# Turning the next pair's key and query groups earlier in a pair of heads, with copies counted head by head and the zero fill in portions

## The chip, the cores and the metric

The kernel runs on one core of one Trainium2 chip. The metric is the device time of one execution in microseconds (us); lower is better. The median of three runs stands for the kernel.

## The reference, cut to what matters

Three stages follow each other: an attention, a mixture of experts with one expert per token, and a gated dense layer. The change lies in the attention alone.

```python
# q, k, v: batch 4, heads 8, sequence 1152, head width 64
q_pool = q.reshape(B, H, S // 2, 2, D).mean(axis=3)          # 576 queries per head
scores = scale * np.matmul(q_pool, k.transpose(0, 1, 3, 2))  # 576 x 1152
scores = scores - np.max(scores, axis=-1, keepdims=True)
attn = np.exp(scores)
attn = attn / (np.sum(attn, axis=-1, keepdims=True) + 1e-09)
attn_out = np.matmul(attn, v)
# then: rows of all heads -> 2304 tokens x 512 -> experts -> dense layer
```

## The kernel before

The attention works on 16 pairs of heads, numbered 0 to 15 (`LAST` is 15). The body of a pair is a list of 27 units, `UNITS`, that every engine walks through in the same order, with one program per engine and semaphores between them. The names of the units: "b" and "c" turn and multiply the probabilities of the pair before (second head, and the rest tile of both heads), "a" those of this pair's first head, "x" turns finished output, and "g" (four groups, g0 to g3) turns keys and summed queries of the **next** pair. Three tables say after which unit the scores, the maxima and the exponentials of each of nine query tiles are placed: `SCORES_AT`, `MAXIMA_AT`, `EXP_AT`. Tile 0 of the next pair is handled at units 24 to 26 of this one.

On PE (TensorE) a unit is first a *fill*, four 128x128 transposes into one of three PSUM banks `ps_t` (L686), and then the *products* of the unit three places earlier (L753, or L762 for "c"). Scores are L784 and, for the last key chunk, L797. The DVE (VectorE) takes the maxima and writes the low part of every turned bank; ACT (ScalarE) writes the high part and the exponentials.

Keys and queries of a pair take this way. SP (SyncE) loads `raw_k` and `raw_q` (L275, L280, L283); POOL (GpSimd) adds the query pairs into `q_sum` (L405, L413); PE turns them in g0 to g3; ACT and DVE write the parts into `kept_rows`; SP copies these by six DMAs, three for each head, into `kq_t` (L295, L296, L298), the operand of the scores. There is one `raw_k`, one `raw_q` and one `parts` buffer, so SP works in a fixed order. Its procedure `next_pair(p)` waits until the DVE has finished g3 of pair p, copies the parts for pair p+1, and then loads keys, queries and values of pair p+2. I call the start of these copies **T(p)**. Before g0 of pair p+1, PE waits for `kq_loaded` and `q_summed` of pair p+2. Before the first scores of a pair it waits for `kq_copied`, which counts all six copies; ACT waits for it too before it overwrites `parts` in g0.

The lines that say this, with SP's order around them:

```python
sp.wait_ge(t_free, upto(p, kind, every, LAST_G))      # next_pair: g3 is done
copy_parts(1 - par)
if load:
    load_kq(p + 2)
    sp.wait_ge(v_split, p + 2)
    load_v(p + 2)
...
pe.wait_ge(kq_loaded, 16 * KQ_DMAS * (p + 2))         # PE, before g0 of pair p
pe.wait_ge(q_summed, 2 * (p + 2))
```

SP also fills with zeros the rows that the expert stage scatters into: `xs_dram` (25 tiles of 128 rows, 6400 KB) and the tail of `ys_dram` (7 tiles, 1792 KB), both before the first `next_pair`.

Of the kernel before, what the change touches and what calls it, by code (L numbers as in the profile page):

```python
# [4 lines left out]
F32 = mybir.dt.float32  # L5
# [7 lines left out]
P = 128  # L13
# [48 lines left out]
def attention(nc, q, k, v, w_gate, w_out_gate, w1, x_dram, xs_dram, ys_dram, shared):  # L62
# [17 lines left out]
    B, H, SK, D = k.shape  # L80
    SQ = SK // 2
    E = w_gate.shape[1]
    PAIRS = B * H // 2
# [31 lines left out]
    ]  # L115
    SCORES_AT = [(25, 26), (0, 1), (2, 3), (6, 7), (10, 12), (12, 14), (16, 16), (19, 20), (22, 23)]
    MAXIMA_AT = [(24, 25), (0, 0), (3, 3), (5, 7), (11, 12), (13, 14), (16, 16), (18, 19), (20, 22)]
    EXP_AT = [(0, 0, 1), (2, 3, 4), (5, 5, 7), (9, 11, 12), (13, 13, 13), (16, 16, 16), (18, 19, 20), (21, 21, 22), (24, 25, 25)]
# [54 lines left out]
    with ctx:  # L173
# [6 lines left out]
        def sem(name):  # L180
            return ctx.enter_context(nc.semaphore(name))
# [30 lines left out]
        ys_zeroed = sem("ys_zeroed")  # L212
# [7 lines left out]
        kq_copied = sem("kq_copied")  # L220
# [21 lines left out]
        KQ_DMAS, X_DMAS, COPIES = 6, 3, 6  # L242
# [26 lines left out]
        with nc.Block() as block:  # L269

            @block.sync
            def _(sp):
# [18 lines left out]
                def copy_parts(par):  # L291

                    for h in range(2):
                        src, at = parts[h * D:h * D + D].bitcast(F32), h * HEAD
                        sp.dma_start(kq_t[par][0:D, at:at + HEAD].bitcast(F32), src[:, 0:LO_K]).then_inc(kq_copied, 16)  # L295
                        sp.dma_start(kq_t[par][D:P, at:at + CH * P].bitcast(F32), src[:, LO_K:LO_K + CH * P]  # L296
                                     ).then_inc(kq_copied, 16)
                        sp.dma_start(kq_t[par][D:P, at + CH * P:at + HEAD].bitcast(F32), src[:, CH * P:LO_K]  # L298
                                     ).then_inc(kq_copied, 16)
# [16 lines left out]
                def next_pair(p, par, kind, load=True):  # L316
# [3 lines left out]
                    if load:  # L320
# [15 lines left out]

                sp.wait_ge(zeros_ready, 1)
                n = xs_dram.shape[0] // P
                sp.dma_start(xs_dram.rearrange("(t p) d -> p t d", p=P),
                             zeros[:, :].rearrange("p (o d) -> p o d", o=1).broadcast_to([P, n, 512])  # L340
                             ).then_inc(x_stored, 16)

                tokens = x_dram.shape[0]
                sp.dma_start(ys_dram[tokens:, :].rearrange("(t p) d -> p t d", p=P),
                             zeros[:, :].rearrange("p (o d) -> p o d", o=1).broadcast_to([P, n - tokens // P, 512])
                             ).then_inc(ys_zeroed, 16)
                next_pair(0, 0, "first")
                with sp.Fori(1, LAST - 2, 2) as p:
                    next_pair(p, 1, "mid")
                    store(p - 1, "mid")  # L350
                    next_pair(p + 1, 0, "mid")
                    store(p, "mid")
                next_pair(LAST - 2, 1, "mid")
# [14 lines left out]
                sp.wait_ge(kq_copied, 16 * COPIES * PAIRS)  # L368
# [4 lines left out]
                sp.wait_ge(ys_zeroed, 16)  # L373
# [109 lines left out]
            def _(act):  # L483
# [6 lines left out]
                def take(p, par, kind, j, step):  # L490
# [4 lines left out]
                    if is_group(step):  # L495
                        if step[1] == 0:

                            act.wait_ge(kq_copied, 16 * COPIES * (p + 1))
                        group_hi(step[1], ring(kind, j))
                        return  # L500
# [182 lines left out]
            def _(pe):  # L683
# [89 lines left out]
                def scores(p, par, tile, h, opening=False):  # L773
# [4 lines left out]
                    if tile == 0 and h == 0:  # L778

                        pe.wait_ge(kq_copied, 16 * COPIES * (p + 1))  # L780
# [1055 lines left out]
```

## Time and profile before

| what | value |
|---|---|
| median of 3 runs | 1724.21 us (1719.8 to 1727.47) |
| the profiled execution, its own time | 1722.07 us |
| its span, first to last instruction | 1720.3 us |
| mean granted TensorE clock | 0.911 of full |
| busy share of the span | PE 83%, PE weight loads 72%, DVE 51%, ACT 37%, POOL 20% |
| end of the attention's last product on PE | 852.5 us from the span's start |

The 1.8 us between span and time lie around the program. The attention takes the first half of the span; the busy shares are averages over stages that differ, so they say little about one of them.

### The profile page before, as it was taken

Reading aid. Unit: us, or ns where it says so; the run is one execution under the profiler, and the core shown is the slowest. Engines: PE = TensorE matmul, PEld = TensorE weight load, DVE = VectorE, ACT = ScalarE, POOL = GpSimd, SP = SyncE. Lnnn points to the kernel's source line nnn. Section 1 sums busy time; section 2 is a strip of 40 time slices with the busy share of each in tenths; the row PEclk is TensorE's granted clock in tenths of the full one; section 3 lists DMA queues with packets and bytes.
Section 4 is the critical chain, followed back from the end, with each engine's and each line's share of the span. In section 5 each row is a group of like instructions: output and inputs, shape, how many; then the busy total and the mean of one; then the engine's idle time right before and its main releaser. Section 6 shows DMA issues by size and latency. Waiting matters only on the chain. (4 is left out here: it accounts for less than half of the span.)

```text
span 1720.3 us, 24853 instructions
## 1 busy us (share of the span) xinstructions
PE 1433.4 (83%) x7733; PEld 1236.4 (72%) x7734; DVE 871.5 (51%) x1658; ACT 639.0 (37%) x1549; POOL 345.1 (20%) x241
## 2 busy tenths in 40 slices
PE   2688777778777778877848988999999999999998
PEld 1567655667655666665636767878789999999998
DVE  1477555667655567656674434444464323323232
ACT  1466555566555466555542133010053111111111
POOL 3011101111101111101078278030130101010000
PEclk7689888889888889888978989999999999999999
DMA  8723444432344432246156356131152001000000
GB/s 208 227 48 75 92 106 106 106 67 65 80 106 106 106 80 65 67 106 182 29 199 240 105 205 219 43 104 37 55 158 87 31 7 38 24 12 18 0 19 19
DMA packets 127738, 156.85 MB, mean 91 GB/s; under 512 B 47440, under 2 KB 86352, under 8 KB 125648
## 3 DMA queue, kind: packets, MB, share of 16 engines
q1 hardware_dynamic: 111776, 114.35, 26.4%
q10 hardware_dynamic: 12880, 31.99, 5.5%
q0 software_dynamic: 3040, 9.96, 1.8%
q8 instruction: 25, 0.41, 0.1%
q14 instruction: 17, 0.14, 0.0%
HBM read 87.33 MB, written 29.10 MB: 68 GB/s over the span
## 5 line engine op out<-in xcount | busy, mean ns | idle before, releaser
L784 PE MATMUL ps_s<-kq_t 128*128 128x512 f32 x640 | 228.7, 455 | 171.0 <-DMA kq_t<-kept_rows 163.9
L570 DVE TENSOR_REDUCE maxima<-ps_s 128x1 f32<-128x512 f32 x288 | 194.7, 685 | 241.3 <-PE ps_s L784 240.9
L506 ACT ACTIVATE p_hi<-ps_t 128x512 fp32r<-128x512 f32 (+1 forms) x336 | 193.6, 584 | 229.2 <-PE ps_t L686 225.2
L784 PEld LDWEIGHTS ps_s<-kq_t 128*128 128x128 f32 x640 | 124.9, 214 | 207.5 <-issue 154.4
L649 DVE TENSOR_TENSOR p_lo<-ps_t,p_hi 128x512 fp32r<-128x512 f32 (+1 forms) x336 | 215.0, 666 | 14.0 <-ACT p_hi L506 9.3
L686 PE MATMUL ps_t<-ident,probs 128*128 128x128 f32 x1296 | 207.5, 286 | 0.0
L686 PEld LDWEIGHTS ps_t<-ident,probs 128*128 128x128 f32 x1296 | 171.8, 149 | 46.6 <-issue 6.3
L530 ACT ACTIVATE probs<-ps_s,neg_max 128x512 f32<-128x512 f32 x288 | 198.5, 689 | 17.5 <-DVE neg_max L583 9.8
L1018 POOL TENSOR_TENSOR w_parts<-raw_w,w_parts 128x1024 fp32r<-128x1024 f32 x64 | 150.8, 2392 | 189.2 <-ACT w_parts L1088 189.0
L1634 ACT ACTIVATE silu<-ps_g 128x384 f32<-128x384 f32 x72 | 35.4, 492 | 314.0 <-PE ps_g L1740 314.0
L753 PE MATMUL ps_o<-p_hi,v_hl 128*128 128x512 f32 x288 | 148.1, 514 | 1.9 <-DVE o_sb L590 1.9
L1088 ACT ACTIVATE w_parts<-raw_w 128x1024 fp32r<-128x1024 f32 x64 | 67.0, 1058 | 220.0 <-PE ps_h L1415 104.3
L1687 DVE TENSOR_TENSOR silu<-ps_g,silu 128x384 f32<-128x384 f32 x72 | 40.1, 557 | 210.1 <-ACT silu L1634 210.1
L753 PE MATMUL ps_o<-p_lo,v_hl 128*128 128x512 f32 x288 | 121.0, 420 | 0.0
L397 POOL TENSOR_TENSOR v_hl<-raw_v,zeros 128x1152 fp32r<-128x1152 f32 x16 | 42.4, 2651 | 318.8 <-PE ps_o L762 295.6
L1738 PE MATMUL ps_g<-mxt_hi,wg 128*128 128x384 f32 x288 | 97.5, 339 | 2.4 <-DVE mxt_lo L1662 2.4
L1740 PE MATMUL ps_g<-mxt_hi,wg 128*128 128x384 f32 x288 | 97.7, 339 | 0.0
L1739 PE MATMUL ps_g<-mxt_lo,wg 128*128 128x384 f32 x288 | 97.3, 338 | 0.0
L1738 PE MATMUL ps_v<-mxt_hi,wv 128*128 128x384 f32 x288 | 96.4, 335 | 0.0
L1739 PE MATMUL ps_v<-mxt_lo,wv 128*128 128x384 f32 x288 | 96.4, 335 | 0.0
L1740 PE MATMUL ps_v<-mxt_hi,wv 128*128 128x384 f32 x288 | 96.4, 335 | 0.0
L1413 PE MATMUL ps_h<-w_parts,xst_hi 128*128 x200 | 82.7, 413 | 14.9 <-POOL w_parts L1018 12.1
(190 smaller groups left out, 2851.8 us busy)
## 6 DMA issues: line engine op xcount, KB each, us to landing
raw_w<-in_moe_w ACTq DMA_DIRECT2D x61, 512.0 KB, 3.6
kq_t<-kept_rows SPq DMA_DIRECT2D x32, 608.0 KB, 6.2
kq_t<-kept_rows SPq DMA_DIRECT2D x32, 320.0 KB, 7.1
raw_k<-in_k SPq DMA_DIRECT2D x32, 288.0 KB, 5.4
raw_v<-in_v SPq DMA_DIRECT2D x16, 576.0 KB, 5.4
kq_t<-kept_rows SPq DMA_DIRECT2D x32, 288.0 KB, 6.5
raw_q<-in_q SPq DMA_DIRECT2D x32, 256.0 KB, 4.1
x_by_slot<-zeros SPq DMA_DIRECT2D x1, 6400.0 KB, 21.6
```

The source lines that it names most:

```text
L506: nc.scalar.activation(p_hi[prob_ring(kind, m)][:, 0:w], T[ring(kind, j)][:, 0:w], ACT.Copy).then_inc(hi_ready, 1)
L530: nc.scalar.activation(probs[:, at:at + 512], S[(2 * tile + h) % SR][:, :], ACT.Exp, bias=neg_max[:, tile:tile + 1], accum_out=sums[par][: ...
L570: nc.vector.reduce_max(maxima[:, 3 * tile + h:3 * tile + h + 1], S[(2 * tile + h) % SR][:, :], AX).then_inc(max_done, 1)
L649: nc.vector.tensor_tensor(p_lo[n][:, 0:w], t[:, 0:w], p_hi[n][:, 0:w].bitcast(F32), ALU.subtract).then_inc(t_free, 1)
L686: last = nc.tensor.transpose(dst[:, n * P:(n + 1) * P], src, ident[:, :])
L753: last = nc.tensor.matmul(O[:, :], v_hl[v_par][:, c * P:(c + 1) * P], part[:, :], start=(i == 0 and n == 0), stop=(i == CH - 1 and n == 1))
L784: last = nc.tensor.matmul(S[(2 * tile + h) % SR][:, :], w, kq_t[par][:, at:at + 512], start=(n == 0), stop=(n == len(ops) - 1))
L1018: nc.gpsimd.tensor_tensor(w_part(n, parity, 1, at, PIECE), raw[j % RAW][:, :], w_part(n, parity, 0, at, PIECE).bitcast(F32), ALU.subtract) ...
L1413: nc.tensor.matmul(HB[h][:, :], xh, dyn(0, base, 0, at), start=(c == 0), stop=False)
L1738: nc.tensor.matmul(dst, wh, xh, start=(c == 0), stop=False)
L1739: nc.tensor.matmul(dst, wh, xl, start=False, stop=False)
L1740: last = nc.tensor.matmul(dst, wl, xh, start=False, stop=(c == DC - 1))
```

## The change

It has four parts. (1) `UNITS` is reordered: g1, g2 and g3 move from places 13, 19 and 20 to 10, 13 and 15; the "x" units and the first "a" units come behind g3. The three tables of tiles are rewritten to go with it. (2) `kq_copied` becomes two semaphores, one for each head; PE waits for the first before tile 0 and for the second before tile 4 (`QT`), ACT still for both. (3) The fill of `xs_dram` is cut into one tile and then two tiles per pair, issued by SP behind each store of the loop; the fill of `ys_dram` follows the loop. (4) The first `next_pair` stands ahead of all zero fill.

```diff
--- before.py
+++ after.py
@@ -110,12 +110,12 @@
 
     UNITS = [
         ("g", 0), ("b", 0), ("b", 1), ("b", 2), ("b", 3), ("b", 4), ("b", 5), ("b", 6), ("b", 7),
-        ("b", 8), ("c", 0), ("c", 1), ("c", 2), ("g", 1), ("x", 0), ("a", 0), ("x", 1), ("a", 1),
-        ("a", 2), ("g", 2), ("g", 3), ("a", 3), ("a", 4), ("a", 5), ("a", 6), ("a", 7), ("a", 8),
+        ("b", 8), ("g", 1), ("c", 0), ("c", 1), ("g", 2), ("c", 2), ("g", 3), ("a", 0), ("a", 1),
+        ("x", 0), ("x", 1), ("a", 2), ("a", 3), ("a", 4), ("a", 5), ("a", 6), ("a", 7), ("a", 8),
     ]
-    SCORES_AT = [(25, 26), (0, 1), (2, 3), (6, 7), (10, 12), (12, 14), (16, 16), (19, 20), (22, 23)]
-    MAXIMA_AT = [(24, 25), (0, 0), (3, 3), (5, 7), (11, 12), (13, 14), (16, 16), (18, 19), (20, 22)]
-    EXP_AT = [(0, 0, 1), (2, 3, 4), (5, 5, 7), (9, 11, 12), (13, 13, 13), (16, 16, 16), (18, 19, 20), (21, 21, 22), (24, 25, 25)]
+    SCORES_AT = [(25, 26), (2, 3), (5, 6), (8, 9), (12, 13), (14, 16), (18, 18), (21, 22), (24, 24)]
+    MAXIMA_AT = [(25, 26), (2, 2), (4, 6), (8, 9), (11, 12), (14, 15), (17, 18), (20, 21), (22, 23)]
+    EXP_AT = [(2, 3, 3), (5, 6, 6), (8, 9, 9), (11, 12, 13), (14, 15, 15), (18, 19, 19), (20, 21, 22), (22, 23, 24), (25, 25, 26)]
 
     assert X_LOADS[X_EARLY - 1][1] * P <= (B - 1) * SQ and (B - 1) * HP <= LAST - 1
     assert w1.shape[2] == PIECE
@@ -209,7 +209,7 @@
         O = ps("ps_o", 512)
 
         zeros_ready = sem("zeros_ready")
-        ys_zeroed = sem("ys_zeroed")
+        rows_zeroed = sem("rows_zeroed")
         kq_loaded = sem("kq_loaded")
         v_loaded = sem("v_loaded")
         pool_chain = sem("pool_chain")
@@ -217,7 +217,7 @@
         q_tiles_summed = sem("q_tiles_summed")
         q_summed = sem("q_summed")
         kq_hi_done = sem("kq_hi_done")
-        kq_copied = sem("kq_copied")
+        kq_copied = [sem(f"kq_copied{h}") for h in range(2)]
         v_split = sem("v_split")
         s_ready = sem("s_ready")
         r_ready = sem("r_ready")
@@ -239,7 +239,7 @@
         v_rows = v.rearrange("b h (p c) d -> (b h) p (c d)", p=P)
         q_rows = q.rearrange("b h (i r) d -> (b h) i (r d)", r=2)
         x_rows = x_dram.rearrange("(b i) (g c) -> b i g c", b=B, g=HP)
-        KQ_DMAS, X_DMAS, COPIES = 6, 3, 6
+        KQ_DMAS, X_DMAS, COPIES = 6, 3, 3
         assert X_DMAS * PAIRS + 1 == X_STORES and x_out.shape[1] == TILES * D
 
         def sum_col(tile, part):
@@ -292,11 +292,12 @@
 
                     for h in range(2):
                         src, at = parts[h * D:h * D + D].bitcast(F32), h * HEAD
-                        sp.dma_start(kq_t[par][0:D, at:at + HEAD].bitcast(F32), src[:, 0:LO_K]).then_inc(kq_copied, 16)
+                        sp.dma_start(kq_t[par][0:D, at:at + HEAD].bitcast(F32), src[:, 0:LO_K]
+                                     ).then_inc(kq_copied[h], 16)
                         sp.dma_start(kq_t[par][D:P, at:at + CH * P].bitcast(F32), src[:, LO_K:LO_K + CH * P]
-                                     ).then_inc(kq_copied, 16)
+                                     ).then_inc(kq_copied[h], 16)
                         sp.dma_start(kq_t[par][D:P, at + CH * P:at + HEAD].bitcast(F32), src[:, CH * P:LO_K]
-                                     ).then_inc(kq_copied, 16)
+                                     ).then_inc(kq_copied[h], 16)
 
                 def store(p, kind):
 
@@ -334,22 +335,27 @@
                 sp.wait_ge(v_split, 1)
                 load_v(1)
 
+                next_pair(0, 0, "first")
+
                 sp.wait_ge(zeros_ready, 1)
-                n = xs_dram.shape[0] // P
-                sp.dma_start(xs_dram.rearrange("(t p) d -> p t d", p=P),
-                             zeros[:, :].rearrange("p (o d) -> p o d", o=1).broadcast_to([P, n, 512])
-                             ).then_inc(x_stored, 16)
-
-                tokens = x_dram.shape[0]
-                sp.dma_start(ys_dram[tokens:, :].rearrange("(t p) d -> p t d", p=P),
-                             zeros[:, :].rearrange("p (o d) -> p o d", o=1).broadcast_to([P, n - tokens // P, 512])
-                             ).then_inc(ys_zeroed, 16)
-                next_pair(0, 0, "first")
-                with sp.Fori(1, LAST - 2, 2) as p:
+                xs_tiles = xs_dram.rearrange("(t p) d -> p t d", p=P)
+                n, tokens = xs_dram.shape[0] // P, x_dram.shape[0]
+                rows = zeros[:, :].rearrange("p (o d) -> p o d", o=1)
+
+                def zero_rows(first, count):
+                    return sp.dma_start(xs_tiles[:, bass.ds(first, count), :], rows.broadcast_to([P, count, 512]))
+
+                zero_rows(0, 1).then_inc(x_stored, 16)
+                with sp.Fori(1, LAST - 3, 2) as p:
                     next_pair(p, 1, "mid")
                     store(p - 1, "mid")
+                    zero_rows(2 * p - 1, 2).then_inc(rows_zeroed, 16)
                     next_pair(p + 1, 0, "mid")
                     store(p, "mid")
+                    zero_rows(2 * p + 1, 2).then_inc(rows_zeroed, 16)
+                assert n == 2 * (LAST - 3) + 1
+                sp.dma_start(ys_dram[tokens:, :].rearrange("(t p) d -> p t d", p=P),
+                             rows.broadcast_to([P, n - tokens // P, 512])).then_inc(rows_zeroed, 16)
                 next_pair(LAST - 2, 1, "mid")
                 store(LAST - 3, "mid")
                 next_pair(LAST - 1, 0, "mid", load=False)
@@ -365,12 +371,13 @@
                                  ).then_inc(shared.raw_loaded[j], 16)
                 store(LAST - 2, "mid")
 
-                sp.wait_ge(kq_copied, 16 * COPIES * PAIRS)
+                for h in range(2):
+                    sp.wait_ge(kq_copied[h], 16 * COPIES * PAIRS)
                 sp.wait_ge(x_stored, 16 * (X_DMAS * (LAST - 1) + 1))
                 for i in range(X_EARLY):
                     shared.load_x(sp, i)
 
-                sp.wait_ge(ys_zeroed, 16)
+                sp.wait_ge(rows_zeroed, 16 * (LAST - 2))
                 store(LAST - 1, "last")
                 store(LAST, "tail")
 
@@ -495,7 +502,8 @@
                     if is_group(step):
                         if step[1] == 0:
 
-                            act.wait_ge(kq_copied, 16 * COPIES * (p + 1))
+                            for h in range(2):
+                                act.wait_ge(kq_copied[h], 16 * COPIES * (p + 1))
                         group_hi(step[1], ring(kind, j))
                         return
                     m = sum(map(is_prob, steps(kind)[:j]))
@@ -775,9 +783,9 @@
                     if not (opening and 2 * tile + h < SR):
 
                         pe.wait_ge(exp_done, 2 * TILES * p + 2 * tile + h - SR + 1)
-                    if tile == 0 and h == 0:
-
-                        pe.wait_ge(kq_copied, 16 * COPIES * (p + 1))
+                    if tile in (0, QT) and h == 0:
+
+                        pe.wait_ge(kq_copied[tile // QT], 16 * COPIES * (p + 1))
                     ops = operands(par, tile)
                     for n, (w, head) in enumerate(ops):
                         at = head * HEAD + h * 512
```

The first place is PE in the loop over the middle pairs, from g3 to g0 of the following pair. `raw_k` and `q_sum` mark the "g" units, `stack,o_sb` the "x" units, `probs` the others; rows of `ps_o` are products. Before, from g3 (row one) on:

```order
L686 MATMUL ps_t<-ident,q_sum 128x128 x2
L753 MATMUL ps_o<-p_hi,v_hl 128x512
L753 MATMUL ps_o<-p_lo,v_hl 128x512
L777 REGISTER_ALU
L784 MATMUL ps_s<-kq_t 128x512 x2
L698 REGISTER_ALU
L686 MATMUL ps_t<-ident,probs 128x128 x4
L753 MATMUL ps_o<-p_hi,v_hl 128x512
L753 MATMUL ps_o<-p_lo,v_hl 128x512
L698 REGISTER_ALU
L686 MATMUL ps_t<-ident,probs 128x128 x4
```

Of the change, from g3 on:

```order
L694 MATMUL ps_t<-ident,q_sum 128x128 x2
L770 MATMUL ps_o<-v_hl,p_hi 128x256
L770 MATMUL ps_o<-v_hl,p_lo 128x256
...
L706 REGISTER_ALU
L694 MATMUL ps_t<-ident,probs 128x128 x4
L785 REGISTER_ALU
L792 MATMUL ps_s<-kq_t 128x512 x2
L706 REGISTER_ALU
L694 MATMUL ps_t<-ident,probs 128x128 x4
...
L725 MATMUL ps_t<-stack,o_sb 128x64 x4
L785 REGISTER_ALU
L792 MATMUL ps_s<-kq_t 128x512 x2
```

So g3 is now followed by two "c" products, both "x" units and a0 to a2 with their scores, which stood ahead of it.

The second place is SP in the loop: what stands between the loads of one pair and the copies of the next (`kept_rows` are the parts). Before:

```order
L288 DMA raw_v<-in_v 128x2x576
L304 REGISTER_ALU
L306 ISA
L308 ISA
L308 DMA x_rows<-x_out 128x4x128
L312 ISA
L312 DMA x_rows<-x_out 64x64
L312 ISA
L312 DMA x_rows<-x_out 64x64
```

And of the change:

```order
L313 ISA
L313 DMA x_rows<-x_out 64x64
L346 ISA
L346 DMA x_by_slot<-zeros 128x2x512
L319 ISA
L295 DMA kq_t<-kept_rows 64x2432
```

One DMA of two tiles of zeros has come in behind the store and ahead of the next pair's wait; nothing stands in a new place between the copies and the loads.

## Rows read from the trace of the kernel before

**Rows 1.** The view of waits, whole span: us in total, times, longest
```profile
PE ps_s L784 <- DMA kq_t<-kept_rows: 163.9, 16, 15.5
PE ps_t L686 <- POOL q_sum L413: 47.4, 16, 10.8
```

**Rows 2.** PE in order of time, one pair: start us, us
```profile
420.46 0.44 PE L686 MATMUL ps_t<-ident,q_sum 128*128 128x128 f32 x2 [0.31 <-DVE p_lo L649]
...
427.31 0.40 PE L753 MATMUL ps_o<-p_lo,v_hl 128*128 128x512 f32 x1
437.55 1.19 PE L784 MATMUL ps_s<-kq_t 128*128 128x512 f32 x2 [9.84 <-DMA kq_t<-kept_rows]
...
444.58 1.03 PE L686 MATMUL ps_t<-ident,raw_k 128*128 128x128 f32 x4 [2.37 <-POOL q_sum L413]
...
471.54 0.44 PE L686 MATMUL ps_t<-ident,q_sum 128*128 128x128 f32 x2 [0.31 <-DVE p_lo L649]
```

**Rows 3.** SP's queue in the same pair: start us, time to issue
```profile
423.45 0.49 SPq L295 DMA_DIRECT2D kq_t<-kept_rows  x1
...
432.99 3.35 SPq L275 DMA_DIRECT2D raw_k<-in_k  x2
...
439.02 0.51 SPq L283 DMA_DIRECT2D raw_q<-in_q  x1
...
474.52 0.50 SPq L295 DMA_DIRECT2D kq_t<-kept_rows  x1
```

**Rows 4.** POOL in the same pair
```profile
442.33 1.41 POOL L405 TENSOR_TENSOR q_sum<-raw_q 128x256 f32<-128x256 f32 x2 [20.67 <-DMA raw_q<-in_q]
```

**Rows 5.** SP's queue: first copies of T(0) and of T(14)
```profile
65.88 0.49 SPq L295 DMA_DIRECT2D kq_t<-kept_rows  x1
...
781.27 0.48 SPq L295 DMA_DIRECT2D kq_t<-kept_rows  x1
```

**Rows 6.** PE in order of time, dense work, for prices from start to start
```profile
457.05 0.60 PE L686 MATMUL ps_t<-ident,probs 128*128 128x128 f32 x4
457.40 0.48 PE L753 MATMUL ps_o<-p_hi,v_hl 128*128 128x512 f32 x1
...
457.95 0.49 PE L686 MATMUL ps_t<-ident,probs 128*128 128x128 f32 x3
...
458.74 0.63 PE L784 MATMUL ps_s<-kq_t 128*128 128x512 f32 x2
459.21 0.49 PE L686 MATMUL ps_t<-ident,probs 128*128 128x128 f32 x3
...
462.98 0.36 PE L762 MATMUL ps_o<-v_hl,p_hi 128*128 128x256 f32 x1
...
463.77 1.00 PE L717 MATMUL ps_t<-stack,o_sb 128*128 128x64 f32 x8
464.58 0.36 PE L762 MATMUL ps_o<-v_hl,p_hi 128*128 128x256 f32 x1
```

**Rows 7.** Windows: stretch, length, busy us of engines, PEclk, DMA share, GB/s
```profile
428.00:433.00 5.00, 0.00 (x0) 0.00 (x0) 0.25 (x1) 1.34 (x5) 0.00 (x0) 0.81 1.02 223
...
444.58:447.82 3.24, 3.24 (x13) 2.74 (x13) 1.16 (x2) 1.62 (x5) 0.00 (x0) 0.52 0.00 0
448.00:471.50 23.50, 23.15 (x152) 19.74 (x151) 20.90 (x46) 18.55 (x50) 4.09 (x2) 1.00 0.00 0
...
795.56:799.11 3.55, 3.55 (x11) 2.88 (x11) 1.29 (x2) 0.60 (x1) 0.64 (x2) 0.50 0.95 292
```

**Rows 8.** PE: g1 of pair 0, and the first scores inside pair 15
```profile
52.66 1.05 PE L686 MATMUL ps_t<-ident,raw_k 128*128 128x128 f32 x4
...
800.24 0.68 PE L784 MATMUL ps_s<-kq_t 128*128 128x512 f32 x2
```

**Rows 9.** The page's DMA issues: KB each, median us to landing
```profile
raw_w<-in_moe_w ACTq DMA_DIRECT2D x61, 512.0 KB, 3.6
...
x_by_slot<-zeros SPq DMA_DIRECT2D x1, 6400.0 KB, 21.6
```

## The prediction

> **What bounds the kernel now.** I read the page's busy tenths first: only the first half of the span, the attention, has an engine pattern that repeats with gaps on every engine, and only there do the edits act. The view of waits then names the gaps: PE waits 163.9 us for the copies of keys and queries and 47.4 us for POOL's query sums, each 16 times [rows 1]. It would be wrong to take the larger number for the price. The order in time shows what is tied to what. In the pair shown, g3 is filled at 420.46, SP starts the copies at 423.45, PE runs dry at 427.71, gets its scores at 437.55, and starts g0 at 444.58, after a second wait of 2.37 us that POOL ends [rows 2, 3]. SP issues the key loads only behind the copies, at 432.99, and the last query load at 439.02 [rows 3]; POOL starts its sums at 442.33, as that load lands [rows 4], and g0 can start 2.25 us later. Then PE works from g0 to the next g3, 444.58 to 471.54, and SP's next copies start at 474.52.
>
> So the pair is one closed chain with three parts:
> - T to g0, copies then loads then sums: 444.58 - 423.45 = 21.13 us
> - g0 to g3, PE's work: 471.54 - 444.58 = 26.96 us
> - g3 to T, the last parts by ACT and DVE: 474.52 - 471.54 = 2.98 us
>
> Together 51.07 us. From T(0) at 65.88 to T(14) at 781.27 there are 14 such rounds of 51.10 us on average [rows 5], so the pair shown is typical. The 9.84 us wait is *inside* the first part. If it alone went away, g0 would still come 21.13 us after T. What counts is how much of PE's work lies within those 21.13 us instead of between g0 and g3.
>
> **The new order, step by step.** g3 moves ahead of work that PE did before it. Prices, at full clock, from start to start [rows 6]: a fill of four transposes 457.40 - 457.05 = 0.35 us; products of an "a" or "b" unit 457.95 - 457.40 = 0.55 us; half a tile of scores 459.21 - 458.74 = 0.47 us; the products of a "c" unit 463.77 - 462.98 = 0.79 us; an "x" fill 464.58 - 463.77 = 0.81 us. By the two `UNITS` lists and score tables, these pass behind g3:
> - both "x" fills: 1.62
> - the fills of a0, a1 and a2: 1.05
> - products of c1 and c2: 1.58
> - products of a0: 0.55
> - four halves of scores, the second of tile 5, both of tile 6, the first of tile 7: 1.88
>
> The sum is 6.7 us. Nothing of weight comes the other way. g0 to g3 shrinks from 26.96 to 20.3 us; the waits between engines in it (the DVE is busy 20.90 of 23.50 us in its dense part [rows 7]) I leave as they are.
>
> **The clock.** The granted clock is already falling within 428 to 433, when PE has been idle since 427.71: the stretch has a mean of 0.81. After the wait PE runs at 0.50 (1.2 of 2.4 GHz) [rows 7]. Before, part of this slow work was done ahead of g0, and behind g0 another 3.24 us of it, at a mean clock of 0.52 [rows 7]. In the new order the idle time lies directly at g0, so all slow work falls between g0 and g3. At T(14) it lasted 3.55 us [rows 7], and covered one fill, the products of one "a" unit and two halves of scores, 1.84 us at full clock: slow work costs about half of its own time. I take 4.3 us of slow work instead of 3.24, that is 0.5 us more per round; the bounds are nothing and 4.65 + 3.24 = 7.9 us of slow work, the most that PE does in the old order from 437.55 on, or 2.3 us more. Here the waits might also have ended differently, so I keep both ends.
>
> **g3 to T.** Before, g2 stood right ahead of g3, and ACT and DVE did the parts of both in a row. Now a "c" unit lies between. I take 2.5 us, with 1.5 (half the old value) and 2.98 as bounds.
>
> **T to g0.** SP's instructions from the copies to the query loads are the same and in the same order, and the DMA engines are full in that time (share 1.02 in 428 to 433 [rows 7]). So 21.1 us stays; bounds 20.5 and 22.
>
> The new round: 21.1 + 20.3 + 0.5 + 2.5 = 44.4 us, 6.7 us less. Fourteen rounds give 93.8 us.
>
> **The two ends.** In pair 0 g3 now stands about where g1 stood, which PE filled at 52.66 [rows 8], ahead of it only short fills. T(0) falls to 52.66 + 2.5 = 55.2 us against 65.88, a gain of 10.7 us. After T(14) there is no load to wait for. Before, pair 15 began with its first scores at 800.24 [rows 8], 19.0 us behind T(14), since PE stood still for the copies. In the new order PE goes on without a stop: 7.25 us of work that followed g3 before (420.46 to 427.71), at most 4.7 us that followed the wait (795.56 to 800.24 [rows 7, 8], 2.7 at full clock) and the 6.7 us moved, with 1 us of small waits, 17.6 us behind g3 or 15.1 behind T. Gain 3.9 us.
>
> **Edits costed at nothing.** The semaphore per head: PE reaches the next pair's tile 0 some 12 us behind T, when three of six copies should have landed; before, all six had landed 14.1 us behind T (437.55 against 423.45 [rows 2, 3]). If it waited for all six it would lose 2 us, but behind it PE waits at g0 anyway, for 21.1 - 15.1 = 6 us. That wait is the cover; without it the shared semaphore would cost those 2 us a pair. ACT waits for both heads at g0, 21 us behind T, later than they land. The zero fill: its large DMA landed after 21.6 us [rows 9] and nothing in the attention waits for it. The portions of 512 KB stand in SP's queue behind loads and store, about 19 us behind T, and the next copies come at 44. A DMA of this size lands in 3.6 us [rows 9], so the cover is 20 us of empty queue. Behind the portion stands SP's wait for the next g3, which it doesn't delay.
>
> The twelve portions of two tiles, one after the other, take 12 x 3.6 = 43 us against 21.6 for the one large DMA [rows 9]; laid on the chain they would cost 3.6 us per round. Here the Trainium skill speaks against the change: "DMA: Bandwidth & Descriptors", section "Bandwidth", asks for at least 1 MiB per DMA, and the page gives a fixed cost of about 2 us for each. By that figure the twelve extra DMAs would cost an estimated 24 us if something waited for them, and the total would come out some 24 us above mine. No row shows such a wait.
>
> **The sum.** 10.7 + 93.8 + 3.9 = 108.4 us, from the profiled execution's 1722.07: 1613.7 us. The median is 2.1 us above that execution, so about 1615 us.
>
> **Rivals.**
> - *Order waits between g0 and g3.* The tables are new, and the DVE has only a tenth of this stretch free. Its 9 halves of scores might each wait 0.4 us more for an exponential: 4 us a round, 56 us in all, 1671 us. For it: DVE busy 20.90 of 23.50. Against it: the waits that the old order shows on PE ahead of g3 are of 0.31 us [rows 2]. 0.13.
> - *PE alone sets the pace.* If T to g0 were short enough, a round would be PE's own time without slow work: 20.3 - 1.5 (half of the 3.24) from g0 to g3, and 17.6 - 2.0 from g3 to g0, 34.4 us. That is 16.7 us less per round, 14 x 16.7 + 14.6 = 248 us, 1474 us. It needs T to g0 under 13 us (15.6 - 2.5); with the DMA share at 1.02 nothing shortens it. A partial gain, from loads that land sooner, lies between. 0.06.
> - *Nothing moves.* The chain keeps its 51.1 us, because the wait reappears whole at g0; only the ends gain 14.6, 1709 us. It would need the g0 to g3 stretch to stay at 27 us with 6.7 us less work in it. 0.03.
> - *The portions lie on the chain.* A portion of 3.6 us ahead of loads or copies, 50 us in all, 1665 us. The queue's order speaks against it. 0.03.
> - *Slower: the clock doesn't come back.* The whole stretch from g0 to g3 runs at 1.2 GHz, 17.4 us of work at full clock (20.3 less 1.5 for the slow part and 1.4 for small gaps) of which 1.8 are slow in any case: 15.6 x 0.93 = 14.5 us more, a round of 58.9, 14 x 7.8 - 14.6 = 95 us more, 1819 us. It decides once more than half of the stretch is slow (7.7 us of extra time per round use up all gains). Against it: soon after the stop in the pair shown the clock was back, 448 to 471.5 ran at 1.00 [rows 7]. 0.03.
>
> **How the numbers follow.** The forecast has 0.72. Its own range: 14 rounds with 43.0 us (2 us of g3 to T, less slow work, 20.5 for T to g0) to 46.7 us give 1595 to 1647. The range for 8 in 10 takes in most of the order waits, and above all a part of the second rival: 1575 to 1662. A difference of under 0.5% (about 8.6 us) is what a measurement of this kernel can't tell from no change. All cases but the last are faster by more: 0.95 faster; 0.02 within, for a "nothing moves" without its ends; 0.03 slower.
>
> **What would show each step.** T(0) near 55 and T(14) near 677 in SP's queue, 44.4 us apart on average. PE's wait for `kq_t` from pair 1 on gone or under 1 us; the wait for `q_sum` grown from about 2.4 to about 6 us, fourteen times. From T to g0 21.1 us, from g0 to g3 near 20.8. A clock of 0.5 behind each g0 for about 4 us. Zero portions issued about 19 us behind T. The stages behind the attention unchanged in length. Wrong would be the prediction if the copies or loads took another time under denser work on the engines, if g0 to g3 held waits for `probs` or for `ps_t` of over 2 us, or if SP came late to the copies behind its portion.

## The result, and the profile after

| | before | changed |
|---|---|---|
| median, us | 1722.01 (1718.59 to 1727.47) | 1605.17 (1603.54 to 1608.19) |
| ratio, 95% interval | 1 | 0.9321 [0.929, 0.9352] |
| profiled execution and its span, us | 1722.07, 1720.3 | 1604.07, 1602.3 |
| mean granted clock | 0.911 | 0.937 |
| T(0), T(14), mean of the 14 rounds, us | 65.88, 781.27, 51.10 | 52.69, 666.60, 43.85 |

The change makes the kernel faster by 6.8%. Of the 118.0 us that the span lost, 65.88 - 52.69 = 13.2 lie ahead of T(0), 14 x 7.25 = 101.5 between T(0) and T(14), and the other 3.3 behind T(14). The attention's last product on PE ends at 734.3 us, where it was 852.5; the stages behind it take 868.0 us of the span, where they took 867.8.

The page's row of busy times: PE has as many instructions as before (7733) and is busy for 88% of the span, where it was 83%.

```profile
PE 1402.7 (88%) x7733; PEld 1220.5 (76%) x7734; DVE 868.0 (54%) x1658; ACT 631.3 (39%) x1549; POOL 345.4 (22%) x241
```

The view of waits on PE, limited to 40 to 700 us (us in total, times, longest). The wait for `kq_t` that headed [rows 1] isn't in it at all; POOL's sums are now PE's one large wait:

```profile
PE ps_t L694 <- POOL q_sum L420: 97.5, 14, 8.3
PE ps_s L792 <- ACT probs L538: 2.9, 4, 0.9
PE ps_o L761 <- DVE o_sb L598: 1.8, 1, 1.8
```

One pair of the changed kernel, to be held against [rows 2, 3]. First PE in order of time (start, length), from g3 of one pair over the scores of the next to g0 and g3 again:

```profile
402.24 0.38 PE L694 MATMUL ps_t<-ident,q_sum 128*128 128x128 f32 x2
...
416.05 0.62 PE L792 MATMUL ps_s<-kq_t 128*128 128x512 f32 x2
...
417.89 1.00 PE L805 MATMUL ps_r<-kq_t 128*128 128x128 f32 x8
...
425.62 1.12 PE L694 MATMUL ps_t<-ident,raw_k 128*128 128x128 f32 x4 [6.73 <-POOL q_sum L420]
...
445.98 0.38 PE L694 MATMUL ps_t<-ident,q_sum 128*128 128x128 f32 x2
```

Then SP's queue in the same pair (start, time to issue), with the first copies of T(0) and T(14) that answer [rows 5]:

```profile
52.69 0.48 SPq L295 DMA_DIRECT2D kq_t<-kept_rows  x1
...
404.40 0.49 SPq L295 DMA_DIRECT2D kq_t<-kept_rows  x1
...
413.90 3.32 SPq L275 DMA_DIRECT2D raw_k<-in_k  x2
...
420.07 0.50 SPq L283 DMA_DIRECT2D raw_q<-in_q  x1
...
423.83 0.44 SPq L346 DMA_DIRECT2D x_by_slot<-zeros  x1
...
448.14 0.49 SPq L295 DMA_DIRECT2D kq_t<-kept_rows  x1
...
666.60 0.48 SPq L295 DMA_DIRECT2D kq_t<-kept_rows  x1
```

The chain is read as before. T is 404.40. The last query load is issued at 420.07, g0 starts at 425.62, 21.22 us behind T; g3 is filled at 445.98, 20.36 later; the next copies start at 448.14, 2.16 later. Together 43.74 us. Over the fourteen rounds the three parts are 21.41, 20.28 and 2.17 us on average. PE gets the scores at 416.05 without a wait and runs dry 6.73 us ahead of g0, at 418.89.

Windows, three stretches of this pair (length, busy us of PE, PEld, DVE, ACT, POOL, granted clock, DMA share, GB/s), to be held against [rows 7]:

```profile
418.87:425.62 6.75, 0.02 (x1) 0.00 (x1) 1.17 (x3) 0.00 (x0) 2.03 (x4) 0.86 1.15 278
425.62:430.72 5.10, 5.10 (x18) 4.37 (x19) 1.38 (x2) 1.65 (x3) 0.00 (x0) 0.51 0.21 78
430.72:445.98 15.26, 15.23 (x97) 12.73 (x96) 14.47 (x30) 13.19 (x37) 0.00 (x0) 1.00 0.00 0
```

PE stands still in the first, works at 1.2 of 2.4 GHz for 5.10 us in the second, and at full clock up to g3 in the third, in which the DMA engines move nothing.

### The profile page after: what moved, and what is told of

The parts are those of the page before. It is cut to its first block and busy times, and to the rows that moved or that the text cites. A ratio compares the mean times of both kernels' runs of the same rounds, so it can differ in the third digit from the quotient of the medians.

```text
span 1602.3 us, 24905 instructions
## 1 busy us (share of the span) xinstructions
PE 1402.7 (88%) x7733; PEld 1220.5 (76%) x7734; DVE 868.0 (54%) x1658; ACT 631.3 (39%) x1549; POOL 345.4 (22%) x241
## 5 line engine op out<-in xcount | busy, mean ns | idle before, releaser
L657 DVE TENSOR_TENSOR p_lo<-ps_t,p_hi 128x512 fp32r<-128x512 f32 (+1 forms) x336 | 218.7, 666 | 35.8 <-ACT p_hi L514 30.2
L792 PE MATMUL ps_s<-kq_t 128*128 128x512 f32 x640 | 204.1, 418 | 13.5 <-DMA kq_t<-kept_rows 9.5
L538 ACT ACTIVATE probs<-ps_s,neg_max 128x512 f32<-128x512 f32 x288 | 199.3, 692 | 17.2 <-DVE neg_max L591 15.1
L694 PEld LDWEIGHTS ps_t<-ident,probs 128*128 128x128 f32 x1296 | 168.5, 147 | 44.1 <-issue 5.7
L792 PEld LDWEIGHTS ps_s<-kq_t 128*128 128x128 f32 x640 | 114.7, 195 | 39.6 <-ACT probs L538 11.1
L694 PE MATMUL ps_t<-ident,raw_k 128*128 128x128 f32 x144 | 32.5, 354 | 117.8 <-POOL q_sum L420 117.8
L694 PEld LDWEIGHTS ps_t<-ident,raw_k 128*128 128x128 f32 x144 | 22.6, 180 | 122.5 <-POOL q_sum L420 99.4
L569 DVE SCALAR_TENSOR_TENSOR kept_rows<-ps_t,kept_rows 128x512 fp32r<-128x512 f32 (+3 forms) x80 | 40.7, 527 | 131.9 <-ACT kept_rows L494 131.5
```

Source lines behind the costliest of these rows:

```text
L538: nc.scalar.activation(probs[:, at:at + 512], S[(2 * tile + h) % SR][:, :], ACT.Exp, bias=neg_max[:, tile:tile + 1], accum_out=sums[par][: ...
L657: nc.vector.tensor_tensor(p_lo[n][:, 0:w], t[:, 0:w], p_hi[n][:, 0:w].bitcast(F32), ALU.subtract).then_inc(t_free, 1)
L694: last = nc.tensor.transpose(dst[:, n * P:(n + 1) * P], src, ident[:, :])
L792: last = nc.tensor.matmul(S[(2 * tile + h) % SR][:, :], w, kq_t[par][:, at:at + 512], start=(n == 0), stop=(n == len(ops) - 1))
```

## Experiments

The theory: a pair is the closed chain of T to g0 (copies, loads and sums in SP's order), g0 to g3 (PE) and g3 to T, and only the length of that chain counts; the order of the units is the whole gain. The rivals: the gain is the vanished wait for `kq_t` (the semaphore of each head), or the zero fill's new place. Kernels were run in three groups of four, each group on one chip beside runs of the kernel before; ratios are to those. The kernel before has a median of 1722.01 us beside the changed kernel and of 1721.42, 1721.74 and 1722.62 in the three groups, so a difference of 2 us between kernels of different groups says little. Mean rounds, T(0) and the waits are read from one profiled execution of each kernel.

### One part undone, one part alone

**e1_one_sem** undoes part 2 in the changed kernel:

```diff
-        kq_copied = [sem(f"kq_copied{h}") for h in range(2)]
+        kq_copied = [sem("kq_copied")] * 2
...
-        KQ_DMAS, X_DMAS, COPIES = 6, 3, 3
+        KQ_DMAS, X_DMAS, COPIES = 6, 3, 6
...
-                    if tile in (0, QT) and h == 0:
+                    if tile == 0 and h == 0:
```

> The changed kernel with one shared semaphore for all six copies again. Closed-chain theory: PE reaches tile 0 of the next pair about 11.7 us behind T and would wait some 2.5 us for the last copy, but its wait at g0 shrinks by as much; the round stays 43.8 us, and only pair 15, which has no g0, pays 2.5 us once. 1605 to 1610 us. Rival, each wait counts by itself: 14 x 2.5 us more, about 1640 us.

Measured: 1607.47 us, 0.9352 [0.9326, 0.9378], mean round 43.66 us. The changed kernel has 1605.17, and the two intervals overlap. PE in one pair of it, the scores of tile 0 and then g0, and the same scores in pair 15:

```profile
415.98 0.70 PE L792 MATMUL ps_s<-kq_t 128*128 128x512 f32 x2 [2.29 <-DMA kq_t<-kept_rows]
...
423.32 1.12 PE L694 MATMUL ps_t<-ident,raw_k 128*128 128x128 f32 x4 [4.44 <-POOL q_sum L420]
...
678.64 1.19 PE L792 MATMUL ps_s<-kq_t 128*128 128x512 f32 x2 [2.35 <-DMA kq_t<-kept_rows]
```

The wait for all six copies is back with 2.29 us, and the wait at g0 has shrunk to 4.44: 6.73 together, as long as the changed kernel's one wait. Two waits in a row on one engine, of which the second ends at a fixed moment, cost no more than one. In other pairs the two waits sum to less, on average to 2.7 + 3.0 = 5.7 us against 7.0, because the clock falls in the first of them: behind the wait of 2.40 us that ends at 460.36, the same scores and units take 4.24 us at a mean clock of 0.66, and 2.90 at 1.00 in the pair shown. The round is no longer for it. Only in pair 15, where no g0 follows, do the 2.35 us cost anything: the attention ends at 736.1 us, 1.8 later than in the changed kernel, though T(14) came 2.2 earlier.

**e2_zero_first** puts the two large zero fills ahead of the first `next_pair` again:

```diff
-                next_pair(0, 0, "first")
-
                 sp.wait_ge(zeros_ready, 1)
...
-                zero_rows(0, 1).then_inc(x_stored, 16)
+                sp.dma_start(xs_dram.rearrange("(t p) d -> p t d", p=P),
+                             zeros[:, :].rearrange("p (o d) -> p o d", o=1).broadcast_to([P, n, 512])
+                             ).then_inc(x_stored, 16)
...
+                next_pair(0, 0, "first")
...
-                    zero_rows(2 * p - 1, 2).then_inc(rows_zeroed, 16)
```

> The changed kernel with the two large zero fills ahead of the first next_pair, as before. Closed-chain theory: rounds unchanged; but T(0) now comes at 52.7 us and the large fills landed near 57 us in the kernel before, so the first copies queue behind them and the first round grows by 4 to 6 us. About 1610 us. Rival, the portions cost time in each round (they land in 4.5 us): 12 x 1 to 4 us faster, 1557 to 1593 us. Rival, the fills have no part in anything: 1605 us.

Measured: 1607.01 us, 0.9339 [0.9324, 0.9355]. T(0) is 53.62 us, the first round 45.4 us against 44.4, the mean round 43.93. The first round's surcharge is 1 us and not 4 to 6, so my expectation of it was too high; and even that isn't clear of the scatter, since e5 below, whose zero fill stands as in the changed kernel, has a first round of 45.4 us too. Nor do the rounds get shorter without the portions. The place of the zero fill is worth about 2 us of the 118 at most.

**e3_heads_alone** is the kernel before with part 2 alone:

```diff
-        kq_copied = sem("kq_copied")
+        kq_copied = [sem(f"kq_copied{h}") for h in range(2)]
...
-                    if tile == 0 and h == 0:
+                    if tile in (0, QT) and h == 0:
 
-                        pe.wait_ge(kq_copied, 16 * COPIES * (p + 1))
+                        pe.wait_ge(kq_copied[tile // QT], 16 * COPIES * (p + 1))
```

> The kernel before with the semaphore per head alone, old tables and old zero fill. Closed-chain theory: PE's wait for the copies falls from 9.8 to 3 to 5 us, its wait at g0 grows by as much, the round stays 51 us, perhaps 0.5 us longer since more slow-clock work falls behind g0: 1715 to 1732 us. Rival, waits add up: 14 x 6 us less, about 1640 us.

Measured: 1717.44 us, 0.9977 [0.9962, 0.9991], mean round 51.22 us (before 51.10). PE in one pair:

```profile
422.29 0.44 PE L688 MATMUL ps_t<-ident,q_sum 128*128 128x128 f32 x2 [0.31 <-DVE p_lo L651]
...
433.43 1.22 PE L786 MATMUL ps_s<-kq_t 128*128 128x512 f32 x2 [3.91 <-DMA kq_t<-kept_rows]
...
446.50 1.12 PE L688 MATMUL ps_t<-ident,raw_k 128*128 128x128 f32 x4 [8.77 <-POOL q_sum L414]
...
473.49 0.44 PE L688 MATMUL ps_t<-ident,q_sum 128*128 128x128 f32 x2 [0.31 <-DVE p_lo L651]
```

This is the plainest evidence of the chain. The wait for `kq_t` fell from 9.84 [rows 2] to 3.91 us, and the wait at g0 rose from 2.37 to 8.77; g0 to g3 is 26.99 us as before. Some 6 us of wait went from one row to the other, and the round stayed. The gain of 4.0 us between the medians is barely clear of noise. In the trace T(14) is 783.73, 2.5 us later than before, and the attention ends at 849.8, 2.8 us earlier: what part 2 gains lies behind T(14), from where the chain isn't closed. The span is 5.6 us shorter, but half of that lies in the later stages, which this edit doesn't touch.

**e4_order_alone** is the kernel before with part 1 alone, the list `UNITS` and the three tables of the changed kernel as in its diff:

```diff
-        ("b", 8), ("c", 0), ("c", 1), ("c", 2), ("g", 1), ("x", 0), ("a", 0), ("x", 1), ("a", 1),
-        ("a", 2), ("g", 2), ("g", 3), ("a", 3), ("a", 4), ("a", 5), ("a", 6), ("a", 7), ("a", 8),
+        ("b", 8), ("g", 1), ("c", 0), ("c", 1), ("g", 2), ("c", 2), ("g", 3), ("a", 0), ("a", 1),
+        ("x", 0), ("x", 1), ("a", 2), ("a", 3), ("a", 4), ("a", 5), ("a", 6), ("a", 7), ("a", 8),
...
```

> The kernel before with the new unit list and tables alone. Closed-chain theory: all of the gain but the two small terms above, 2.5 us for pair 15 and 4 to 6 us for the first round: about 1612 us (1606 to 1618). Rival, a good part of the gain comes from the semaphore or from the zero fill: over 1640 us.

Measured: 1607.49 us, 0.9349 [0.9333, 0.9365], T(0) 52.60, T(14) 666.38, mean round 43.84 us. T(14) is within 0.2 us of the changed kernel's. So the order of the units, with its tables, is the whole gain up to there; list and tables weren't taken apart. Behind T(14) e4 still has a wait of 2.36 us for `kq_t` in pair 15, and its attention ends at 738.0, 3.7 us later than in the changed kernel. That is what parts 2 to 4 bring together in these two traces; the spans (1604.3 and 1602.3) differ by 2.0 us, which is within the intervals.

### What sets T to g0

After the change 21 of 44 us are T to g0, and PE stops for 6.7 of them. Four kernels ask which part of it can be shortened, and a fifth follows from their answers.

**e5_two_parts** gives the parts of odd and even pairs a buffer each (`kept_rows` and the other half of that space, `x_half`), so that ACT needn't wait for this pair's copies before it overwrites them:

```diff
-        parts = shared.x_half[0][:, 0:LO_K + CH * P].bitcast(F32R)
+        parts = [half[:, 0:LO_K + CH * P].bitcast(F32R) for half in shared.x_half]
...
-                                act.wait_ge(kq_copied[h], 16 * COPIES * (p + 1))
+                                act.wait_ge(kq_copied[h], 16 * COPIES * p)
```

> The changed kernel with a second buffer for the parts, so that ACT at g0 no longer waits for the copies of the same pair. Theory: T to g0 is bound by the loads behind the copies and by POOL's sums, not by that wait; nothing changes, rounds 43.8 us, 1605 us. Rival, ACT's wait for both heads holds the chain too: rounds below 43 us.

Measured: 1607.42 us, 0.9334 [0.9303, 0.9366], mean round 43.93 us. No change: this buffer isn't in the chain as long as the copies stand ahead of the loads.

**e6_loads_first** is the changed kernel with the loads of keys and queries issued ahead of the copies:

```diff
                     sp.wait_ge(t_free, upto(p, kind, every, LAST_G))
-                    copy_parts(1 - par)
                     if load:
                         load_kq(p + 2)
+                    copy_parts(1 - par)
...
```

> The changed kernel with SP issuing the key and query loads ahead of the six copies; one parts buffer. Theory: the sums are ready about 9 us behind T and g0 is free of them; head 0 lands near T + 14, so PE waits about 2 us at tile 0, and ACT must wait at g0 for all copies, near T + 20, by which time PE has done three more units. A round of 38 to 40 us, 1530 to 1550 us. If the chain from T to g0 did not bind, rounds would stay near 43.8 us.

Measured: 1533.45 us, 0.8889 [0.8848, 0.893], mean round 38.57 us. On PE the wait for sums is gone from 40 to 640 us, and this is left for the copies, which now come later:

```profile
PE ps_s L792 <- DMA kq_t<-kept_rows: 30.7, 14, 3.5
```

**e7_parts_h0_loads_h1** has both buffers of e5 and issues head 0's copies, the loads, then head 1's copies; **e8_h0_loads_h1** has the same order with one buffer:

```diff
-                    copy_parts(1 - par)
+                    copy_parts(1 - par, (0,))
                     if load:
                         load_kq(p + 2)
+                    copy_parts(1 - par, (1,))
...
```

> Two parts buffers, and SP's order head 0's copies, loads, head 1's copies. Theory: the sums are ready near T + 15.6, when PE gets to g0 at T + 14.5, and nothing else waits for head 1; the round is PE's own work with small waits, 35 to 37 us, and the total 1490 to 1510 us. Rival, denser DMA and engine work lengthen the round: 39 us or more, over 1535 us.

> As the last one but with one parts buffer. Theory: ACT waits at g0 for head 1's copies until T + 20; PE goes on for three units; a round of 38 to 40 us, about 1540 us, so that the second parts buffer is worth 2 to 4 us a round here though nothing in the order of the changed kernel.

Measured: e7 1510.68 us, 0.8757 [0.8715, 0.8799], mean round 37.06; e8 1533.41 us, 0.8895 [0.8861, 0.8929], mean round 38.92. The view of waits says what each waits for, first e7 and then e8:

```profile
PE ps_t L695 <- POOL q_sum L421: 24.9, 14, 2.9
```

```profile
ACT kept_rows L495 <- DMA kq_t<-kept_rows: 75.9, 14, 6.9
```

The buffer that was worth nothing in e5 is worth 23 us here: with head 1's copies behind the loads, ACT waits for them in g0. e7 ends just past the slow edge of its expectation; PE still waits 24.9 / 14 = 1.8 us a pair for the sums.

**e9_loads_at_fill** follows from that: two buffers, and the loads issued as soon as PE has *filled* g3 (which is when `raw_k` and `q_sum` are read for the last time), not when the DVE has finished with it; the copies follow at T, all behind the loads. These are two edits at once. The diff is against e7.

```diff
-                    sp.wait_ge(t_free, upto(p, kind, every, LAST_G))
-                    copy_parts(1 - par, (0,))
                     if load:
+                        sp.wait_ge(t_filled, upto(p, kind, every, LAST_G))
                         load_kq(p + 2)
-                    copy_parts(1 - par, (1,))
+                    sp.wait_ge(t_free, upto(p, kind, every, LAST_G))
+                    copy_parts(1 - par)
```

> Two parts buffers, and SP issues the key and query loads as soon as PE has filled g3 (some 2 us before T), then all copies at T. Theory: the sums end 7 to 9 us behind T, head 0 lands near T + 11, just as PE gets to tile 0 at T + 11.7; nothing of the chain is left on PE's way. Rounds 35 to 36.5 us against 37.1 in the version with head 0, loads, head 1, and 1488 to 1505 us. Rival: rounds stay at 37, since PE's own order waits or slower DMAs under load set them; 1511 us.

Measured: 1484.28 us (1477.56 to 1488.92), 0.8609 [0.8583, 0.8636], mean round 35.09 us: the fastest version, 121 us faster than the changed kernel, and a little faster than expected. SP's queue in one pair, and a window over a whole round:

```profile
337.49 1.43 SPq L275 DMA_DIRECT2D raw_k<-in_k  x2
...
341.62 0.51 SPq L283 DMA_DIRECT2D raw_q<-in_q  x1
342.18 0.59 SPq L295 DMA_DIRECT2D kq_t<-x_half  x1
...
372.42 1.43 SPq L275 DMA_DIRECT2D raw_k<-in_k  x2
```

```profile
337.00:372.00 35.00, 34.90 (x229) 29.82 (x227) 32.56 (x68) 28.66 (x80) 7.34 (x6) 1.00 0.60 145
```

PE is busy 34.90 of 35.00 us at full clock. This is the second rival of the prediction, PE alone sets the pace, which gave a round of 34.4 and 1474 us. Its price was about right; what it needed was another order in SP's queue and a second buffer for the parts. How much of the 26 us against e7 the earlier wait brings, and how much the place of the copies, wasn't tried apart.

### The same edits in the kernel before

**e10_before_loads_first** is the edit of e6 in the kernel before; **e11_before_heads_loads_first** adds the semaphores of e3 to it. Both have

```diff
-                    copy_parts(1 - par)
                     if load:
                         load_kq(p + 2)
+                    copy_parts(1 - par)
...
```

> The kernel before, with SP's loads ahead of the copies and nothing else. Theory: the old order has tile 0 of the next pair ahead of g0 on PE, only 4 us behind T, and it waits for all six copies, which now land near T + 20; g0 follows 4.7 us later. A round of 53 us, about 1750 us: slower, though the same edit made the changed kernel 72 us faster. Rival, the loads are what the chain waits for in either order: rounds below 50 us, under 1700 us.

> As the last one, with a semaphore per head as well. Theory: tile 0 now waits for head 0 alone, until T + 14, and g0 follows at T + 18.5; rounds of 47 to 48.5 us, about 1675 us. So the semaphore per head, worth 4 us in the old SP order, is worth 70 to 80 us in this one.

Measured: e10 1743.7 us, 1.0114 [1.0081, 1.0146], mean round 52.10; e11 1657.51 us, 0.9634 [0.9604, 0.9663], mean round 46.64 (a little shorter than expected). PE in one pair of e10, then the loads in SP's queue:

```profile
401.30 1.19 PE L784 MATMUL ps_s<-kq_t 128*128 128x512 f32 x2 [14.96 <-DMA kq_t<-kept_rows]
...
405.93 0.63 PE L686 MATMUL ps_t<-ident,raw_k 128*128 128x128 f32 x4
...
431.23 0.44 PE L686 MATMUL ps_t<-ident,q_sum 128*128 128x128 f32 x2 [0.31 <-DVE p_lo L649]
```

```profile
382.25 1.43 SPq L275 DMA_DIRECT2D raw_k<-in_k  x2
...
434.38 1.44 SPq L275 DMA_DIRECT2D raw_k<-in_k  x2
```

The edit that took 72 us from the changed kernel costs the kernel before 21 us. Its chain is another one: from SP's start to the first scores 401.30 - 382.25 = 19.05 us, 4.63 to g0, 25.30 to g3, 3.15 to SP's next start, 52.13 in all. Here the wait for `kq_t` *is* in the chain, and so the semaphore per head, worth 4.0 us in SP's old order (e3, 1721.42 before and 1717.44; 1.5 to 6.5 by its interval), is worth 1743.7 - 1657.5 = 86 us.

### The price of a portion of zeros

**e12_zeros_on_chain** puts each of the twelve portions between copies and loads, where the chain waits for it, and takes it from behind the stores:

```diff
                     copy_parts(1 - par)
+                    if zero is not None:
+                        zero_rows(zero, 2).then_inc(rows_zeroed, 16)
                     if load:
...
-                    zero_rows(2 * p - 1, 2).then_inc(rows_zeroed, 16)
```

> The changed kernel with each portion of two zero tiles between a pair's copies and its loads, in the twelve pairs of the loop. Theory: the portion takes the DMA engines for 512 KB in a full queue, 1.8 to 2.5 us a round, which all shows in T to g0: 1627 to 1636 us. Rival by its landing time of 4.5 us: 1659 us. Rival, the chain doesn't bind: 1605 us.

Measured: 1627.87 us, 0.9458 [0.9433, 0.9484], mean round 45.43 us. SP's queue in one pair:

```profile
417.58 0.49 SPq L295 DMA_DIRECT2D kq_t<-kept_rows  x1
...
427.14 1.64 SPq L348 DMA_DIRECT2D x_by_slot<-zeros  x1
428.99 3.62 SPq L275 DMA_DIRECT2D raw_k<-in_k  x2
...
463.49 0.49 SPq L295 DMA_DIRECT2D kq_t<-kept_rows  x1
```

The loads start 11.41 us behind T, against 413.90 - 404.40 = 9.50 in the changed kernel: 1.9 us. The total says the same, (1627.87 - 1605.17) / 12 = 1.9 us per portion. A portion that the chain has to let pass costs 1.9 us, about half of the 3.6 us that the rival with the portions on the chain charged. In e12 the portions landed after 6.5 us (median), so the landing time isn't the price either. The prediction's estimate of 24 us is near the 22.7 us measured. It rests on the fixed cost of about 2 us per DMA in the Trainium skill ("DMA: Bandwidth & Descriptors", section "Anatomy of one DMA — SWDGE (gpsimd) path"), which is given there for DMAs that GpSimd issues, while the portions are issued by SP. The measurement doesn't confirm that reason: 512 KB at the 278 GB/s of the window above take 1.9 us too, so bytes alone can explain it, and no run tells the two apart. Off the chain, in the changed kernel, the portions cost nothing that e2 and e4 could show.

## Why the prediction was right, point by point

It forecast 1615 us and 108.4 us of gain; measured are 1605.17 and 118.0 in the span. Of the 9.6 us between, the rounds have 7.7, T(0) 2.5, and the end -0.6. Within a round the three parts missed by +0.3, -0.5 and -0.3 us, partly against each other, so that the sum is a little better than its terms.

- *"the pair is one closed chain with three parts"*, and the 9.84 us wait is inside it. Shown, by e3 (the wait moved, the round stayed) and e1, and by e10, where the same wait got into the chain.
- *T to g0, 21.1 us*: measured 21.22 in the pair shown and 21.41 on average; the first three rounds have 21.9, 22.8 and 21.9.
- *g0 to g3, 20.3 and 0.5 for the clock*: measured 20.36, on average 20.28, the largest miss within a round. The list of what moves was right, its price of 6.7 us too low. In the rows of before, the moved work is all that PE did from 463.77 [rows 6] to g3 at 471.54 [rows 2] but for the 0.35 us of g2's fill at 470.16: 7.4 us. The last half of scores took 1.03 us there, with the wait of 0.31 us for the DVE, where I charged 0.47, and some fills and scores a little more than their price. The clock cost more too: the 5.10 us of slow work (I took 4.3) are three fills and three products, 2.7 us at full clock, so 2.4 us were lost; before, from 444.58 to 448.51, 3.93 us of work that takes 2.27 at full clock, 1.7 lost. So 26.96 - 7.4 + 0.7 = 20.3 us. The rows of before:

```profile
448.51 0.63 PE L784 MATMUL ps_s<-kq_t 128*128 128x512 f32 x2
...
470.16 0.27 PE L686 MATMUL ps_t<-ident,raw_k 128*128 128x128 f32 x1
470.27 0.49 PE L686 MATMUL ps_t<-ident,q_sum 128*128 128x128 f32 x3
470.51 0.71 PE L784 MATMUL ps_s<-kq_t 128*128 128x512 f32 x2
```

- *g3 to T, 2.5*: measured 2.16, inside the bounds of 1.5 and 2.98.
- *The new round of 44.4*: measured 43.85 on average, 43.74 in the pair shown.
- *T(0) at 55.2*: mis-sized by 2.5 us, the larger of the two misses at the ends. I put g3 of pair 0 where g1 had stood, at 52.66 [rows 8]. It is filled at 50.66, and T follows 2.03 us later. The zero fill's place has no clear part in it: e4, with all of it in front, has T(0) at 52.60, e2 at 53.62. Of the 2 us by which PE comes earlier, 0.9 are there at g0 of pair 0 already (36.70 where it was 37.62); what brings them wasn't tried alone. PE's row of the fill:

```profile
50.66 0.38 PE L694 MATMUL ps_t<-ident,q_sum 128*128 128x128 f32 x2
```

- *End behind T(14), 3.9*: measured 3.3 in the span and 3.5 up to the attention's last product. *The stages behind the attention unchanged in length*: 867.8 and 868.0 us.
- *The wait for `kq_t` gone, that for `q_sum` grown to about 6 us, fourteen times*: 6.73 in the pair shown, 97.5 us over 14 times between 40 and 700 us, 7.0 on average. PE ran dry 14.5 us behind T, not 15.1: from g3 at 402.24 on it worked 16.65 us without a stop, and the 1 us of small waits that I had put into the 17.6 didn't come.
- *The semaphore per head covered by the wait at g0*, "without it the shared semaphore would cost those 2 us a pair": e1 shows the 2 us (2.29) and the cover. The case without cover is e10 against e11, where it isn't 2 but 5.5 us a round (52.10 against 46.64), because there the copies come behind the loads.
- *The zero fill at nothing, portions some 19 us behind T*: issued at 423.83, 19.4 behind T. Landing took 4.5 us, where I had 3.6 [rows 9]; the page's row of DMA issues:

```profile
x_by_slot<-zeros SPq DMA_DIRECT2D x12, 512.0 KB, 4.5
```

- *Order waits*: didn't come. In the part of g0 to g3 at full clock the DVE is busy 14.47 of 15.26 us, nearly all the time, and PE still 15.23.
- *Slower, the clock doesn't come back*: it was back 5.10 us behind g0.
- *"with the DMA share at 1.02 nothing shortens it"*, said of T to g0 against the second rival: true of the order of SP's queue as it stood, wrong as a reason. e9 moves the same bytes and comes within 11 us of the rival's time, because the loads needn't stand behind the copies.

## What to carry to other kernels

Where buffers and a fixed queue tie a pair of a loop to the next, write down the closed chain with its parts before pricing any wait: PE's largest wait (163.9 us) was worth next to nothing by itself (e3 took 6 of its 10 us a pair away, and the round stayed), and the work that lay on the wrong side of the chain's last wait was worth 7 us a pair. An edit has no price of its own; the loads ahead of the copies gave 72 us with one order of units and cost 21 with the other, and the semaphore per head was worth 4 or 86 us. When a chain ends in a transfer, ask which event really frees its target (here the fill, not the last reader of its result) and try its issue there.

## What the runs showed of the hardware

- The two loads of `raw_k` took 3.3 us to issue when the copies stood ahead of them in the queue (413.90 above) and 1.43 us when SP's last issue was 15.8 us back (e9, 337.49). So of the 3.3 us, 1.9 come with the copies ahead of the loads, and not with the loads themselves.
- The landing time of a portion isn't its price: it landed in 4.5 us behind a store and in 6.5 on the chain (medians), and cost 1.9 us there.
- After a stop of 6.7 us PE worked 5.10 us at a granted clock of 0.51 (1.2 GHz), and then at 1.00. So a stop of 6.7 us costs more than 6.7: 2.4 us besides, by the prices of [rows 6].
- A stop of 2.3 us can bring the clock down, or not: in e1 PE worked at 1.00 behind the wait of 2.29 us that ends at 415.98, and at a mean of 0.65 for 4.28 us behind another of 2.29 us that ends at 634.32. What decides it, no run shows.
- The mean granted clock of the profiled executions is 0.911 before, 0.937 with the change and 0.967 in e9, where PE hardly stops in the attention; over all executions it is 0.908 to 0.926, 0.937 to 0.943 and 0.967 to 0.981.
